# A three-stage kernel (attention, experts, feed-forward): the feed-forward takes its rows in the order of the experts

## What is computed

```python
# 1. attention, local (|i-j| < 4) plus a pooled one
x = attn_out.transpose(0, 2, 1, 3).reshape(2304, 512)
# 2. top-1 experts: E = 8, F = 1024
logits = (x / |x|) @ (emb / |emb|).T / tau
expert_idx = argmax(logits, axis=1)
gate_w = softmax(logits)[arange(N), expert_idx]
for e in range(8):
    mask = expert_idx == e
    h = maximum(x[mask] @ w1[e], 0.0)
    out[mask] = gate_w[mask, None] * (h @ w2[e])
# 3. feed-forward, 512 -> 2048 -> 512
h = x @ w_in
g = maximum(0.01 * h, h)
return g @ w_out
```

## Time and profile before

| | us |
|---|---|
| median of 3 runs | 932.9 |
| lowest, highest | 930.83, 936.19 |
| the profiled execution | 931.14 |
| its span in the trace | 929.3 |

### The profile page before, as it was taken

How to read it: one execution, slowest core, us unless ns; L and a number is a source line. 1 busy time by engine, 2 the same in 40 slices (tenths; PEclk the granted TensorE clock), 3 DMA queues, 4 the chain that set the end, 5 groups by cost and what they waited for, 6 DMA issues and landing times.

```text
span 929.3 us, 17237 instructions
## 1 busy us (share of the span) xinstructions
PE 875.5 (94%) x5872; PEld 736.1 (79%) x5878; DVE 535.9 (58%) x783; ACT 519.2 (56%) x930; POOL 141.6 (15%) x230
## 2 busy tenths in 40 slices
PE   8898986899999999999993999999999999999997
PEld 4787773677777778777773888898889899898896
DVE  5677754788988898888883544223223223223222
ACT  3677783788887888888874453232232233233222
POOL 7675772010110110100003000001001001000000
PEclk9999999999999999999996999999999999999999
DMA  8586576352726744611102000100100101100000
GB/s 220 167 235 201 186 233 242 109 208 100 295 80 244 266 147 194 271 59 35 35 23 60 20 1 10 59 1 13 55 0 17 50 0 29 38 0 29 6 1 34
DMA packets 45083, 92.35 MB, mean 99 GB/s; under 512 B 3912, under 2 KB 23208, under 8 KB 40944
## 3 DMA queue, kind: packets, MB, share of 16 engines
q1 hardware_dynamic: 36896, 48.20, 16.6%
q0 software_dynamic: 8144, 43.57, 12.4%
HBM read 72.96 MB, written 18.79 MB: 99 GB/s over the span
## 4 chain that ended last, share of the span: by engine, by line
PE 80%; DVE 5%; ACT 5%; issue 4%; DMA 2%; POOL 2%; SPq 1%; DVEq 0%; ACTq 0%; POOLq 0%
PE banks L826 68%; PE banks L764 2%; PE banks L858 2%; ACT ehi L1075 1%; PE banks L907 1%; PE banks L742 1%; PE banks L669 1%; DVE elo L1385 1%; DVE xTlo L1390 1%; PE banks L706 1%; PE banks L718 1%; PE banks L677 1%; PE banks L833 1%; PE banks L736 1%; ACT pdin L978 1%
## 5 line engine op out<-in xcount | busy, mean ns | idle before, releaser
L1385 DVE TENSOR_TENSOR elo<-wslot,ehi 128x1024 fp32r<-128x1024 f32 x196 | 237.6, 1224 | 37.8 <-ACT ehi L1075 29.2
L1075 ACT ACTIVATE ehi<-wslot 128x1024 fp32r x196 | 204.9, 1059 | 45.3 <-PE banks L826 37.8
L1475 DVE SCALAR_TENSOR_TENSOR fg<-fraw 128x384 f32<-128x384 f32 x96 | 53.6, 558 | 216.3 <-ACT fraw L1164 216.3
L1164 ACT ACTIVATE fraw<-banks 128x384 f32<-128x384 f32 x96 | 47.2, 492 | 227.1 <-PE banks L826 227.1
L826 PE MATMUL banks<-zhi,winhi 128*128 (+1 forms) x384 | 131.5, 342 | 1.2 <-DVE zlo L1468 1.2
L826 PE MATMUL banks<-zhi,winlo 128*128 (+1 forms) x384 | 130.0, 339 | 0.0
L826 PE MATMUL banks<-zlo,winhi 128*128 (+1 forms) x384 | 129.5, 337 | 0.0
L826 PE MATMUL banks<-wouthi,fhi 128*128 128x512 f32 x288 | 113.2, 393 | 3.4 <-DVE flo L1480 3.4
L826 PE MATMUL banks<-wouthi,flo 128*128 128x512 f32 x288 | 113.9, 396 | 0.0
L826 PE MATMUL banks<-woutlo,fhi 128*128 128x512 f32 x288 | 113.6, 394 | 0.0
L826 PE MATMUL banks<-ehi,xThi 128*128 128x512 f32 x200 | 83.1, 415 | 6.5 <-DVE xTlo L1390 6.5
(11 more groups left out here) (193 smaller groups left out, 1362.4 us busy)
## 6 DMA issues: line engine op xcount, KB each, us to landing
wslot<-in_w POOLq DMA_DIRECT2D x24, 1024.0 KB, 9.1
wslot<-in_w SPq DMA_DIRECT2D x8, 1024.0 KB, 6.1
xr<-xs SPq DMA_DIRECT2D x25, 272.0 KB, 2.8
ys<-y_sb SPq DMA_DIRECT2D x25, 256.0 KB, 2.0
qb<-in_qT SPq DMA_DIRECT2D x16, 288.0 KB, 4.0
kb<-in_kT SPq DMA_DIRECT2D x16, 288.0 KB, 6.1
vq<-in_vtok SPq DMA_DIRECT2D x32, 144.0 KB
out_x<-o_sb SPq DMA_DIRECT2D x6, 768.0 KB, 4.4
```

Of the source, the lines that this page charges most:

```text
L1075: act.activation(ehi[:, ring_at(k), :], wslot[:, chunk_cols(offs[dt], matrix, half, c)], ACT.Copy).then_inc(s_ehi, 1)
L1164: act.activation(fraw[:, f % 2, :], banks[:, f % 2, 0:TB], ACT.Copy).then_inc(s_fhev, 1)
L1385: dve.tensor_tensor(elo[:, ring_at(k), :], wslot[:, chunk_cols(offs[dt], matrix, half, c)], ehi[:, ring_at(k), :].bitcast(F32), ALU.subtra ...
L1475: dve.scalar_tensor_tensor(out=fg[:, f % 2, :], in0=fraw[:, f % 2, :], scalar=0.01, in1=fraw[:, f % 2, :], op0=ALU.mult, op1=ALU.max).then ...
```

## The change

The feed-forward takes the sorted rows as they lie in `ys`, with the padding of the last tile of each expert skipped: rank r of the sorted order instead of token r.

- Two lists are computed on DVE: for each rank its row in `ys`, and for each token its rank (`rank_at`, `rank_i`). This and the gates' computation stand ahead of the experts' tiles on DVE and ACT. POOL fills a small table of numbers at the start (`riota`).
- Gate and token number of each token, 8 bytes, are scattered by POOL to the DRAM tensor `gates` at the token's rank: 18 indirect DMAs, nine behind the weight loads of expert 2 and nine behind those of expert 3. Behind those of expert 4 the table is loaded back as `row_gate`.
- Sorted order lets a gather run ahead: block b's rows lie in the first 3(b+1) + 7 tiles of `ys`. Blocks 0 and 1 are gathered by POOL behind the last weight load; `yg` has a place of its own in SBUF.
- In the last expert tile PE transposes block 0's rows into four banks, ACT and DVE round them and the first three weight chunks of the feed-forward there.
- The gate is the scale factor of the eviction to `o_sb`; `gate_rows` is gone. DVE's two evictions wait for ACT's and for each other.
- The output is scattered: three indirect DMAs of 256 KB per block on POOL, in place of one of 768 KB on SP.

```diff
--- before.py
+++ after.py
@@ POOL, constants
+                gp.iota(riota_i[:], pattern=[[NQ, NTOK]], base=0, channel_multiplier=1)
...
+                gp.tensor_copy(riota[:], riota_i[:])
+                gp.tensor_copy(tok_gate[:, :, 1], riota_i[:])
@@ POOL, experts
+            def put_gates(t0, t1):
+                if t0 == 0:
+                    gp.wait_ge(s_rank_at, 1)
+                    gp.wait_ge(s_tok_gate, 1)
+                for t in range(t0, t1):
+                    gp.indirect_dma_start(gates, bass.IndirectOffsetOnAxis(rank_i[:, 1, t:t + 1], 0),
+                                          tok_gate[:, t, :], None).then_inc(s_gput, 16)
...
+                if e == SLOTS:
+                    put_gates(0, NTOK // 2)
+                if e == SLOTS + 1:
+                    put_gates(NTOK // 2, NTOK)
+                if e == SLOTS + 2:
+                    gp.wait_ge(s_gput, 16 * NTOK)
+                    gp.dma_start(row_gate[:], gates.rearrange("(t p) c -> p t c", p=NQ)).then_inc(s_gget, 16)
                 gp.wait_ge(s_wl[e % SLOTS], 64 * (e // SLOTS))
                 gp.sem_inc(s_w, 1)
@@ POOL, feed-forward
-            gp.wait_ge(s_ys, 16 * NT + 16)
...
+            def gather(blk):
+                ready = min(NT, TT * (blk + 1) + E - 1)
+                gp.wait_ge(s_ys, 16 * ready + 16)
+                if blk:
+                    gp.wait_ge(s_zt, KC * blk)
+                for i in range(TT):
+                    t = blk * TT + i
+                    gp.indirect_dma_start(yg[:, i, :], None, ys[0:ready * P, :],
+                                          bass.IndirectOffsetOnAxis(rank_i[:, 0, t:t + 1], 0)).then_inc(s_g, 16)
+            def scatter_out(blk):
+                for i in range(TT):
+                    gp.wait_ge(s_oev, TT * (blk + 1) + i + 1)
+                    t = blk * TT + i
+                    gp.indirect_dma_start(out, bass.IndirectOffsetOnAxis(row_tok[:, t:t + 1], 0),
+                                          o_sb[:, i, :], None).then_inc(s_out, 16)
+            gather(0)
+            for blk in range(NB):
+                if blk + 1 < NB:
+                    gather(blk + 1)
+                scatter_out(blk)
@@ PE, last tile
+                if last:
+                    pe.wait_ge(s_g, 16 * TT)
+                    for k in range(KC):
+                        turn_z(0, k, FIRST_Z[k])
@@ ACT, last tile
+                    act.wait_ge(s_fw, 32 * (E - SLOTS))
+                    act.wait_ge(s_elo, chunk_no(t, 0))
+                    round_chunk(0, 0)
+                    round_chunk(0, 1)
+                    round_chunk(1, 0)
                     round_h(t, 1)
+                    act.wait_ge(s_ed, chunk_no(t, 2 * HC - 1) + 1 + RING)
+                    for k in range(KC):
+                        act.wait_ge(s_zt, k + 1)
+                        act.activation(zhi[:, 0, k, :], banks[:, FIRST_Z[k], 0:TB], ACT.Copy).then_inc(s_zhi, 1)
@@ ACT, block
-                    if f == NF // 2 and not last:
-                        gate_rows(blk + 1)
...
-                act.activation(o_sb[:, 0, :], banks[:, 5, :], ACT.Copy).then_inc(s_oev, 1)
+                act.activation(o_sb[:, 0, :], banks[:, 5, :], ACT.Copy, scale=row_scale(blk, 0)).then_inc(s_oev, 1)
@@ DVE, last tile
+                    rest_of_chunk(0, 0, 1)
+                    rest_of_chunk(0, 1, 2)
+                    rest_of_chunk(1, 0, 3)
                     rest_of_h(t, 1)
+                    for k in range(KC):
+                        dve.wait_ge(s_zhi, k + 1)
+                        dve.tensor_tensor(zlo[:, 0, k, :], banks[:, FIRST_Z[k], 0:TB], zhi[:, 0, k, :].bitcast(F32),
+                                          ALU.subtract).then_inc(s_zlo, 1)
@@ DVE, block
                 for i in (1, 2):
-                    dve.tensor_copy(o_sb[:, i, :], banks[:, 5 + i, :]).then_inc(s_oev, 1)
+                    dve.wait_ge(s_oev, TT * (blk + 1) + i)
+                    dve.tensor_scalar(o_sb[:, i, :], banks[:, 5 + i, :], row_scale(blk, i), None, ALU.mult)\
+                        .then_inc(s_oev, 1)
```

More of the change, by code:

```diff
@@ L614, in _ @@
                 gp.sem_inc(s_w, 1)
-            gp.wait_ge(s_ys, 16 * NT + 16)
-            def gather(blk, first):
-                if not first:
-                    gp.wait_ge(s_zt, KC * blk)
-                gp.tensor_copy(gidx[:], ypos[:, bass.ds(blk * (TB // NQ), TB // NQ)]).then_inc(s_gidx, 1)
-                gp.wait_ge(s_gidx, blk + 1)
-                gp.sem_inc(s_go, 1)
-                for i in range(TB // NQ):
-                    gp.indirect_dma_start(yg[:, i, :], None, ys,
-                                          bass.IndirectOffsetOnAxis(gidx[:, i:i + 1], 0)).then_inc(s_g, 16)
-                gp.wait_ge(s_g, 16 * (TB // NQ) * (blk + 1))
@@ L872, in project, with turn_z @@
                         m.then_inc(s_ed, 1)
+            XB2, OB = (2, 3), (5, 6, 7)
+            def turn_z(blk, k, bank):
+                for i in range(TT):
+                    m = pe.transpose(banks[:, bank, i * NQ:(i + 1) * NQ], yg[:, i, k * P:(k + 1) * P], ident[:])
+                m.then_inc(s_zt, 1)
             def tile(t, at, last):
@@ L915, in first_product @@
                     pe.wait_ge(s_wlo, IN_AT[f])
+                if f == 1 and split:
+                    pe.wait_ge(s_yev, NT + 1)
                 pe.wait_ge(s_fhev, blk * NF + f + 1)
@@ L1398, in load_tile, with rest_of_chunk @@
                 return dve.value_load(slot_i[0:1, bass.ds(t, 1)], min_val=0, max_val=(SLOTS - 1) * 2 * WE)
+            def rest_of_chunk(which, f, n):
+                hi, lo, raw = ((winhi, winlo, winraw), (wouthi, woutlo, woutraw))[which]
+                dve.wait_ge(s_whi, n)
+                dve.tensor_tensor(lo[:, f, :], raw[:, f, :], hi[:, f, :].bitcast(F32), ALU.subtract)\
+                    .then_inc(s_wlo, 1)
             def tile(t, off, last):
```

169 lines of the change are left out of this document (77 added, 92 removed).

## The result

Four runs of each kernel on one chip: 922.6 us after (921.53 to 923.67), 932.2 us before (930.83 to 936.19); the ratio is 0.989, with a 95% interval of 0.9857 to 0.9923. The kernel is faster, and its time lies 1.1 us above the range forecast. The profiled execution took 922.41 us with a span of 920.6 us; its forecast was 915.5 with a span of 913.7. So 6.9 us are to be explained. Some executions of a kernel fall into a slower state, and every ratio here is of the others alone.

A forecast was written before the change was run, and what follows sets the result against it. PE was taken to bound the kernel outside the passage at 490 to 514 us, a serial chain inside it. Span 929.3 - 16.9 - 0.8 + 2.1 = 913.7; time forecast 916.4 us, range 912.5 to 921.5.

The forecast's parts named there:

- The last tile and the first steps: Last expert tile to block 0's first second product: gather, gate, transposes and roundings leave the chain; mark at 497.1, saving 16.9 us.
- Block 0: First feed-forward block: without `gate_rows` PE's hole at its second product goes, saving 0.8 us.
- Between blocks: Handover between feed-forward blocks: evictions in a row end at 581.4 instead of 580.7, ahead of the next work; cost nothing.
- The end: After the last product: three POOL scatters replace one DMA, the last landing at 931.3 instead of 929.3; 2.1 us later.
- The landing: Part of the end's term: a scatter lands 4.3 us behind its start in the median (3.3 to 6.6).
- Ahead of the experts: Before the first expert tile: DVE's extra 5.4 us chain uses 1.5 of 3.97 us idle; cost nothing.
- POOL in the experts: Scatters of 8-byte rows behind POOL's weight loads end at 211.5 to 216.1, before ACT asks at 221.9; cost nothing.
- rivals 1 and 2: POOL's indirect DMAs block DVE fully (chance 0.05), or partly (923) or DVE's front chain exceeds 7.9 us (918; chance 0.09).
- Rival 1: In the experts, 24 indirect DMAs block DVE: 933.7 us at 0.96 each, 944.8 at 1.42; chance 0.05.
- Rival 3: The clock doesn't hold: PE runs block 0's first two first products at half clock, 919 us; chance 0.08.

## Where the prediction was right and where it was wrong

- **The last tile and the first steps: right.** Project at 488.34 (forecast 488.8), first product at 491.51 (491.85), `fraw` at 493.87 (494.15), mark at 496.82 (497.1), clock 1.00 throughout. DVE was the later of the two, as forecast, and the transposes took 1.47 us in the gap of PE, of which 1.76 us were left behind them. The runs with later transposes and later gather show which parts carry the 17 us.
- **Block 0: right.** 69.04 us to the next mark, without the hole at f = 8.
- **Between blocks: wrong by 0.6 us.** "So this costs nothing; it would begin to cost if an eviction with the gate took over 1.2 us each" reckoned with 0.60 and 0.65 us and no time between. They took 0.69 and 0.75 with 0.13 to 0.18 of waiting in between, and in block 1 the last one ran until 0.42 us behind the end of `fraw`, on the engine that the next step needs. The limit of 1.2 us was too high as well: from 579.42 three equal evictions reach DVE's next work at 582.0 once each takes 0.86 us. Side by side, the 0.6 us are gone.
- **The end: the step that failed.** "Now ACT's eviction ends at 924.17, and POOL can issue the first scatter 0.3 us later" and the two issues behind it held (measured from the last product's end: 1.0, 2.3 and 3.5 us). The sum then stopped at the landing and took it for the end of the span. Behind it stood POOL's drain, 7.9 us, which the kernel before had under cover at 793 us. It was in the records of before, though in none of the views that the sum was made from; the step from "SP is last" to "POOL is last" moved it onto the path.
- **The landing, in the same term: 1.6 us too long.** 4.3 us came from the scatters to `xs`, which ran among other traffic; here each landed 2.7 us behind its start. The Trainium skill (DMA: Bandwidth & Descriptors, Anatomy of one DMA — SWDGE (gpsimd) path) gave an estimate of 2.6 us, and the trace agrees with it. The two errors in this term, 7.9 and a further 0.4 behind the landing less 1.6, make 6.7 us.
- **Ahead of the experts: right.** The first `hThi` came at 168.93 (169.25 before).
- **POOL in the experts, and rivals 1 and 2: the result right, the danger put in the wrong place.** The scatters took 0.95 to 1.70 us, `elo` 1224 ns as before. "Over 2.4 us each PE would begin to wait" took the signal for expert 2's weights to stand behind the scatters; it was given at 210.16, before the last two of them, and with two scatters in place of each of the nine, 2.9 us a pair, it came 15.7 us ahead of the train's end. PE did wait in that profile, but for another signal. Rival 1's limit comes out at 0.85 us each (15.6 + 4.8 over 24), not 0.83; nothing hangs on it. The Trainium skill (SBUF — State Buffer, Who interferes with whom) let it expect that descriptor generation escapes the blocking; the runs agree, with DVE at 1224 ns beside twice as many issues; it was POOL's own issues that got longer, 0.95 to 1.85 us.
- **Rival 3: not in the profile of the changed kernel,** where the clock stayed at 1.00 here; but it is not refuted for every execution. In the profile without the drain, with the same instructions up to this place, the clock was at half from 494.0 to 497.4, over the last `project` and not over the first products, and it cost 1.5 us where the rival had priced 3.6. With the late gather it fell for longer, from 500.6 to 510.9.
- **Not seen as a rival at all:** something at the end that none of the busy times counts.

## What to carry to other kernels

Before the last work of a program is given to another engine, ask what that engine still has to do once its work is done, and look for it in the raw records of the kernel before, where it may lie under cover. If POOL must be last, drain it once while it has nothing to do: here that gave 7.6 us for one instruction. And the order in which POOL's program is written did not tell when its signals went out: look for the signal itself in the records before a wait is priced by what stands ahead of it.

## What the runs showed of the hardware

- POOL's drain behind software DMAs: 0.3 us with 3 of them, 0.53 with 6, 6 to 8 us with 73 to 110, 5.05 with 128. Where it was the last thing in the program, no engine worked in that time and DMAs were busy 0.00 to 0.01 of it.
- POOL's signals ran ahead of its DMA issues: the one for expert 2 stood at 210.16, while scatters written ahead of it started until 212.69; with twice as many at 221.74 and 236.49.
- An indirect scatter of 256 KB to the output, with nothing beside it, landed 2.7 us behind its start of 0.96 us; among other transfers those of 272 KB to `xs` took 3.3 to 6.6.
- The kernel before took 932.2, 931.5, 938.4, 938.5 and 933.4 us in five sets of runs, and the profiles differ by single stretches of 3.4 to 10.2 us at half clock; a gain of 1 us is only to be had from stretches of a profile.
